# Attention two units at a time inside a fused attention, feed-forward and routed-experts kernel

## The reference, cut to what matters

```python
def _attn_ref(q, k, v, n_global, n_local):        # 4 batches, 8 heads, 768 positions, head size 64
    scores = scale * np.matmul(q, k.transpose(0, 1, 3, 2))
    keep = is_global | is_local                   # 8 global keys and the last 96
    scores = np.where(keep, scores + bias, -1e9)  # bias: -slope of the head * distance
    a = np.exp(scores - np.max(scores, axis=-1, keepdims=True))
    a = a / (np.sum(a, axis=-1, keepdims=True) + 1e-09)
    return np.matmul(a, v)

def _moe_ref(x, w_in, w_out):                     # x 3072x512, w_in 512x2048, w_out 2048x512
    h = x @ w_in
    return (h * (1.0 / (1.0 + np.exp(-h)))) @ w_out
```

## Time and profile before

| | us |
|---|---|
| median of 3 runs (1129.77 to 1133.5) | 1132.96 |
| the profiled execution | 1131.58 |
| its span, first to last instruction | 1129.9 |
| busy in it: TensorE / VectorE / ScalarE / GpSimd | 1083.3 / 650.0 / 461.6 / 418.4 |

### The profile page before, as it was taken

One profiled execution on the slowest core, in us unless ns is written; L12 is line 12 of the kernel. 1 busy time (PEld: TensorE's weight loads), 2 busy tenths in 40 slices (PEclk: granted clock), 3 DMA queues, 4 the chain that ended last, 5 costly groups with the idle time before them and its releaser, 6 DMA issues. The chain is left out here.

```text
span 1129.9 us, 21205 instructions
## 1 busy us (share of the span) xinstructions
PE 1083.3 (96%) x7992; PEld 906.0 (80%) x7992; DVE 650.0 (58%) x2219; ACT 461.6 (41%) x1167; POOL 418.4 (37%) x472
## 2 busy tenths in 40 slices
PE   7999999999999999999999999947899999999998
PEld 5688888888888888888888888946778777878987
DVE  5766747565655656564747473446757757756110
ACT  3665444444444444444444443202233333333442
POOL 1154222222222222222222222316477565486873
PEclk7799999999999999999999999967999999999999
DMA  6664212111112111212121000005045233433520
GB/s 201 186 200 130 73 53 72 53 48 44 70 54 69 48 67 51 71 54 72 54 72 54 36 20 19 1 19 177 26 181 177 104 126 118 171 111 127 200 103 28
DMA packets 19145, 99.99 MB, mean 88 GB/s; under 512 B 2800, under 2 KB 2800, under 8 KB 16848
## 3 DMA queue, kind: packets, MB, share of 16 engines
q0 software_dynamic: 9824, 58.99, 14.8%
q1 hardware_dynamic: 9216, 39.61, 10.7%
HBM read 86.00 MB, written 12.85 MB: 87 GB/s over the span
## 5 line engine op out<-in xcount | busy, mean ns | idle before, releaser
L346 POOL TENSOR_TENSOR g_low<-g,g_high 128x256 fp32r<-128x256 f32 x192 | 149.4, 780 | 483.2 <-ACT g_high L538 483.2
L443 PE MATMUL up_ps<-x_high,w_high 128*128 128x256 f32 x768 | 224.4, 292 | 0.0
L443 PE MATMUL up_ps<-x_low,w_high 128*128 128x256 f32 x768 | 214.7, 280 | 0.0
L443 PE MATMUL up_ps<-x_high,w_low 128*128 128x256 f32 x768 | 214.3, 279 | 0.0
L676 DVE SCALAR_TENSOR_TENSOR g<-g,up_ps 128x256 f32<-128x256 f32 x192 | 80.6, 420 | 213.3 <-ACT g L531 213.3
L443 PEld LDWEIGHTS up_ps<-x_high,w_high 128*128 128x128 f32 x768 | 144.6, 188 | 27.6 <-issue 21.6
L456 PE MATMUL down_ps<-w_high,g_high 128*128 128x512 f32 x384 | 152.4, 397 | 1.0 <-POOL g_low L346 0.9
L456 PE MATMUL down_ps<-w_high,g_low 128*128 128x512 f32 x384 | 152.3, 396 | 0.0
L456 PE MATMUL down_ps<-w_low,g_high 128*128 128x512 f32 x384 | 152.1, 396 | 0.0
L538 ACT ACTIVATE g_high<-g 128x256 fp32r<-128x256 f32 x192 | 80.2, 418 | 171.4 <-PE down_ps L456 115.8
L665 DVE CUSTOM_DVE_ANT_0 product<-x,w_raw 128x512 f32<-128x512 f32 x176 | 147.3, 837 | 3.0
(11 more groups left out here) (196 smaller groups left out, 1934.7 us busy)
## 6 DMA issues: line engine op xcount, KB each, us to landing
qk_t<-qk_rows SPq DMA_DIRECT2D x24, 720.0 KB, 4.8
v_w<-v_win SPq DMA_DIRECT2D x24, 464.0 KB
w_raw<-weights SPq DMA_DIRECT2D x16, 512.0 KB, 4.5
x_rest<-x_any POOLq DMA_DIRECT2D x24, 256.0 KB, 4.8
x_rows<-x POOLq DMA_DIRECT2D x12, 512.0 KB, 3.2
w_raw<-gate_rows SPq DMA_DIRECT2D x1, 2048.0 KB, 13.8
x_g<-x_rows,token_index POOLq DMA_INDIRECT x24, 3.6
out<-y,token_index POOLq DMA_INDIRECT x24, 2.7
```

Of the source, the lines that this page charges most:

```text
L346: pool.tensor_tensor(g_low[:, u % 2, :], g[:, u % 2, :], g_high[:, u % 2, :].bitcast(F32), ALU.subtract)\
L443: last = nc.tensor.matmul(up_ps[:, u % 2, 0:GT * P], a[:, f, w], x[:, grp % 2, c, :], start=k == 0, stop=k == 3 * C - 1)
```

## The change

From step 12 on, attention is done in pairs of units. In an even step `n` TensorE first runs `score(n)`, `score(n+1)`, `value(n-2)`, `value(n-1)` with nothing between them, and then the chunks. The turns are no longer at the head of a step: `turn(n)` stands behind the second chunk of the even step, `turn(n+1)` behind the first chunk of the odd step, where nothing else of attention is left. The other engines follow: VectorE and ScalarE do `shift`, `exp` and `scale_probs` of both units in the even step, ahead of the chunks; `keep_turned` follows the turns. The end of a row (`replace_x`, `round_x`, `rest_x`) moves from three steps behind the row's last `score` to one step.

Buffers: `probs` has two slots instead of three (a third one of the lead borrows `x2`), `probs_t` has two instead of one, the second unit's scores lie at column 256 of the same banks, `product` (an output of the `dot`s that nobody reads) becomes bf16, and `x2_t` moves to `qk_t`.

Lead: `unread_products` are 10, 3, 3 and 2 in steps 0 to 3 (before: 9, 3, 0, 0). In step 11 the turns of units 10 and 11 and `value(9)` stand behind the two `up`s, and the splits of weights behind them are spread over the two chunks.

```diff
-        probs = sb("probs", [P, 3, 2, window])
+        probs = sb("probs", [P, 2, 2, window])
-        probs_t = sb("probs_t", [P, 4, P])
+        probs_t = sb("probs_t", [P, 2, 4, P])
-        product = sb("product", [P, DM])
+        product = sb("product", [P, DM], BF16)
...
+        def scored_in(n):
+            return [u for u in (n, n + 1) if unit_there(u)] if n >= LEAD and n % 2 == 0 else []
+
+        def valued_in(n):
+            return [u for u in (n - 2, n - 1) if unit_there(u)] if n >= LEAD and n % 2 == 0 else []
+
+        def turned_behind(m):
+            n, k = LEAD + m // 2, m % 2
+            u = n if n % 2 == 0 else n - 1
+            if n < LEAD:
+                return None
+            if n % 2 == 0 and k == 1:
+                return u if unit_there(u) else None
+            if n % 2 == 1 and k == 0:
+                return u + 1 if unit_there(u + 1) else None
+            return None
...
+        def scores_of(u):
+            at = 256 if u >= LEAD and u % 2 else 0
+            return qk_ps[:, :, at:at + keys_of(u // PAIRS)[1]]
...
                 if n < LEAD:
+
+
                     score(n)
-                    unread_products({0: 9, 1: 3}.get(n, 0))
-
-                turn_last = n < LEAD and (n - 3) % PAIRS != 0
-                if unit_there(n - 2) and not turn_last:
-                    turn(n - 2)
-                if unit_there(n - 3):
-                    value(n - 3)
-                if unit_there(n - 2) and turn_last:
-                    turn(n - 2)
-                if n >= LEAD and unit_there(n):
-                    score(n)
+                    unread_products({0: 10, 1: 3}.get(n, 0))
...
+                    unread_products({2: 3, 3: 2}.get(n, 0))
+                for u in scored_in(n):
+                    score(u)
+                for u in valued_in(n):
+                    value(u)
                 for m in chunks_of(n):
                     if chunk_there(m + AHEAD):
                         up(m + AHEAD)
                     if chunk_there(m):
                         down(m)
+
+                    if m == -2:
+                        turn(LEAD - 2)
+                        value(LEAD - 3)
+                    if m == -1:
+                        turn(LEAD - 1)
+                    if turned_behind(m) is not None:
+                        turn(turned_behind(m))
```

More of the change, by code:

```diff
@@ L375, in score @@
                     pe.wait_ge(qk_in[row % 2], 16 * (row // 2 + 1))
-                reached(pe, scores_ready, 2 * u)
+                reached(pe, scores_ready, 2 * (u if u < LEAD else u - u % 2))
                 for a in range(2):
                     part = slice(a * D, (a + 1) * D)
-                    last = nc.tensor.matmul(qk_ps[:, a, 0:width], qk_t[part, row % 2, pair, 0:P],
+                    last = nc.tensor.matmul(scores_of(u)[:, a, :], qk_t[part, row % 2, pair, 0:P],
                                             qk_t[part, row % 2, pair, P:P + width], start=True, stop=True)
@@ L407, in value @@
                         last = nc.tensor.matmul(o_ps[a * D:(a + 1) * D, pair, :], v_w[0:part, row % 2, pair, a, c, :],
[L408 removed]
+                                                probs_t[0:part, u % 2, a * 2 + c, :], start=c == 0, stop=c == 1)
                 last.then_inc(values_done, 1)
@@ L548, in _ @@
                     exp(n, (0,))
-                if unit_there(n - 2):
-                    keep_turned(n - 2)
-                if n < LEAD:
+                    if n >= 2:
+                        keep_turned(n - 2)
                     exp(n, (1,))
-                row = row_ended(n, 3)
+                for u in scored_in(n):
+                    exp(u)
+                row = x_row_in(n)
                 if row is not None:
                     round_x(row)
-                if n >= LEAD and unit_there(n):
-                    exp(n)
                 for f in split_in(n):
-                    round_w(f)
+                    if n != LEAD - 1:
+                        round_w(f)
                 for m in chunks_of(n):
+                    if n == LEAD - 1:
+                        round_w(split_in(n)[m % 2])
                     if chunk_there(m + AHEAD):
                         half_tanh(m + AHEAD)
+                    if m == -2:
+                        keep_turned(LEAD - 2)
                     if chunk_there(m + AHEAD):
                         round_g(m + AHEAD)
+                    if m == -1:
+                        keep_turned(LEAD - 1)
+                    if turned_behind(m) is not None:
+                        keep_turned(turned_behind(m))
                     if m % FC == FC - 1 and chunk_there(m):
@@ L684, in _ @@
                     shift(n)
-                row = row_ended(n, 3)
+                for u in scored_in(n):
+                    shift(u)
+                row = x_row_in(n)
                 if row is not None:
                     replace_x(row)
-                if unit_there(n - 1):
+                if 1 <= n < LEAD:
                     scale_probs(n - 1)
@@ L691, in _ @@
                     rest_x(row)
-                if n >= LEAD and unit_there(n):
-                    shift(n)
+                if n == LEAD - 1:
+                    scale_probs(n)
+                for u in scored_in(n):
+                    scale_probs(u)
                 for f in split_in(n - 1 if n < LEAD - 1 else n):
```

38 lines of the change are left out of this document (27 added, 11 removed).

## The result

| | before | after |
|---|---|---|
| median of the runs | 1132.31 us (4 runs, 1129.77 to 1133.5) | 1113.58 us (4 runs, 1111.81 to 1114.72) |
| ratio, 95% interval | | 0.9836 (0.9813 to 0.9859) |
| profiled execution, its span | 1131.58, 1129.9 us | 1112.91, 1111.3 us |
| first `up` starts | 45.10 us | 40.52 us |
| fused stage, first `up` to last `down` | 693.95 us | 678.94 us |

The change gains 18.7 us in the medians and 18.6 between the two spans: 4.6 ahead of the first `up`, 15.0 in the fused stage, and 0.9 are lost behind it.

The account below looks back on a forecast made before the run. TensorE, busy for 96% of the span, was taken as the bound, so gains come only from losses between its products. 1131.58 - 23.4 (pairs) + 0.5 (burst) + 1.0 (lead) = 1109.7 us, range 1102 to 1119.

Parts of the forecast that it names:

- main term: Fused stage: a pair of units pays 0.55 us of shape-change losses once instead of twice; with the edges -23.4 us.
- cold lead: Forecast case: TensorE's clock stays at half in the lead, added unread products cost about +1.0 us; chance 0.52.
- burst on VectorE: Even steps: both units' VectorE work ahead of the chunks delays `up` slightly in the first group; +0.5 us, range -1 to +3.
- the products themselves are the same: Fused stage: TensorE's products stay unchanged apart from added unread ones, so no term for their rate.
- (a): A turn in front of an `up` loses nothing: taken as 0; other end 0.20 at each of 84 turns, 16.8 us.
- the 0.22 that was named as a sign of being wrong: First `up` product behind a turn: taking 0.22 us instead of its own rate would show the prediction wrong.
- the turns pay too: Rival: a turn between `down` and `up` is also a change of shape, 16.8 us come back, 1126.5 us; chance 0.06.
- (b): A pair's second score might not have its weights loaded ahead: 0 to 0.11 us at 42 places; taken as 0.
- (c): `product` as bf16: no reader and off the path, so 0.
- the chain becomes the bound: Rival: VectorE's queued scalings and `dot`s delay `up(m+4)` in even steps; 1132 to 1160 us; chance 0.10.
- the margin of 1.3 us: Worst even step at a row's end: `twice_silu` ends at 6.8 us, `up(m+4)` wants to start at 8.1.
- warm lead: Rival: denser work brings the full clock back early in the lead, -5 us, total 1103.7 us; chance 0.27.

Follow-up runs that it names:

- e7: Changed kernel with the second scaling moved behind the first `twice_silu` in steps 12 to 17, plus 64 unused bytes ahead of `x_rest`: 1111.34 us, single run.
- e6: Kernel before with only its SBUF layout changed: 192 unused bytes ahead of `x_rest`, `product` as bf16, so `x_high` lies at the changed kernel's address: 1139.46 us, single run.
- e2: Changed kernel with the pieces of an even step ordered score, value, score, value: 1134.33 us, ratio 0.9984 to the kernel before.
- e1: Changed kernel with the second unit's scaling behind the first `twice_silu` in the weight-splitting steps 12 to 17: 1113.16 us, ratio 0.9781 to the kernel before.
- e3: Kernel before with the changed kernel's unread products in the lead (10, 3, 3, 2): 1134.69 us, ratio 0.9967 to the kernel before.
- e4: Changed kernel with the unread products of the kernel before (9, 3, none, none): 1119.99 us, ratio 0.9831 to the kernel before.
- e5: Changed kernel itself, unchanged, repeated on another chip: 1117.55 us, ratio 0.983 to the kernel before.
- e11: Changed kernel itself, unchanged, repeated on another chip: 1119.78 us, ratio 0.9846 to the kernel before.
- e8: Changed kernel with the second scaling moved behind the first `twice_silu` in steps 12 to 17, plus 96 unused bytes ahead of `x_rest`: 1114.17 us, single run.
- e10: Changed kernel where GpSimd's `rest_w` waits for VectorE's `rest_w` in even steps 12, 14, 16: 1119.13 us, single run.

## Why the prediction was right

The forecast was 1109.7 us, a gain of 21.9, with a range of 1102 to 1119; the gain came out 3.2 us smaller. The direction and the mechanism of the main term held. That the whole came out so near is luck: two larger errors, 5.3 us one way and 5.6 the other, cancelled. The signs that the prediction gave itself for being wrong came up: `up` waits for VectorE in even steps of the first group, and the granted clock of 16 to 40 us is another. The time fell into the range of the cold lead (1106 to 1115) with a lead that was warm. The terms, on the profiled executions:

| term | forecast | measured |
|---|---|---|
| 42 pairs and the edges | -23.4 | -21.0 (42 x 0.492 = 20.7; edges 0.35, the remainder of the stage) |
| `up` at 1.417 in the last chunks, without attention | 0 | +0.3 |
| burst on VectorE | +0.5 | +5.8 |
| lead | +1.0 | -4.6 |
| behind the stage | 0 | +0.9 |
| sum | -21.9 | -18.6 |

**Main term: right in kind, 2.4 us too large.** Losses of 0.55 a pair were saved as 0.492. Of the 0.058 missing, 0.014 (e7, in after's order) to 0.032 (e6, in before's) is the place of the operands, 0.6 to 1.3 us in 42 pairs: the step "the products themselves are the same" took their rate for granted, and e6 and e7 show that it is not. The other 0.026 to 0.044 is little more than reading starts to 0.01 us, and (a), the turn in front of an `up`, leaves: turn and `up` together take 0.35 + 1.503 against 0.428 + 1.417, so 0.01 a turn, and 0.03 in e7. The first product of `up` behind a turn does take 0.20 (118.78 to 118.98), nearly the 0.22 that was named as a sign of being wrong, but the turn hands over after 0.35 instead of 0.43, so nothing is lost in the sum. The value chosen there, 0 of 0.20, was right within 0.03, and with it *the turns pay too* falls. A pair was to take 14.25 and took 14.288. (b) was 0 as taken: two scores 0.984, not 1.09. (c) too: the `dot`s got shorter, 138.9 us instead of the 147.3 of the earlier trace rows, off the path. "Issue" idle time of the loads of `up` fell from the 21.4 of the earlier trace rows to 7.4; with the loads of scores and values it fell from 51.3 to 33.0 (48 to 745 us), which is less than the half that was foretold. e2 gives the control: two changes of shape more a pair, 0.355 us more, where the prediction's own pieces give 0.36.

**The burst: the mis-sized term, +0.5 for +5.8.** e1 without the waits gains 6.66; less the 0.9 of waits that before had, that is 5.8. The step that failed is the row of VectorE's work in the first group: it took the scaling at 0.9 from the earlier trace rows and put "a `rest_w` behind them" at its undisturbed time, and asked only what stood in VectorE's own queue. What GpSimd did at that moment was left out, though the trace of before had a GpSimd split of 2.4 us in every step there, and already showed what it does to VectorE: `inv` takes 0.70 instead of 0.17 and ends with it, and the scaling behind it, at 58.40, takes 1.31 beside a `g_low` of GpSimd.

```profile
55.74 2.40 POOL L333 TENSOR_TENSOR w_low<-w_raw,w_high 128x1024 fp32r<-128x1024 f32 x1 [3.58 <-ACT w_high L512]
57.47 0.70 DVE L620 TENSOR_SCALAR inv<-sums 128x2 f32<-128x2 f32 x1
```

TensorE did not wait for it there. In after, scaling and split take 2.68 and 3.40 in GpSimd's company. With these the same sum gives 8.4 + 2.1 = 10.5 against the 8.1 at which `up` wants to start, a wait of 2.4; measured 2.16. The prediction even named the mechanism, under *the chain becomes the bound*, as "`dot`s that get slower beside GpSimd's `rest_g`", and looked at the wrong pair of instructions: the `dot`s were not slower. From 100 us on the margin of 1.3 us held. The 2.2 us left of the 6.7, which fit the low clock behind the waits, had no term in the sum.

**The lead: the choice of cold was wrong.** Its argument ("five products are 2 us of work") measured the products by their length. e3 and e4 show that they lift the clock for the whole lead and are worth 4.0 and 4.2 us, and that a lead at full clock is then held by VectorE, ScalarE and `v_w`. The rival *warm lead* had -5 for this and measured -4.6; with the other terms as forecast it would have been 1103.7, and the waits took that back. The rule from the Trainium skill, page TensorE: Matmul & The Clock Gate (Part 4), by which the prediction gave this rival support, pointed the right way; that transposes as such do not count is not isolated by any run here.

**Behind the stage**: 929.6 to 933 us at the low clock, in work that the change doesn't touch. It varies from run to run: e5 and e11, the same kernel, have three and two such stretches at other times. So nothing here shows the 0.9 as an effect of the change.

## What to carry to other kernels

When work is moved on one engine, look at what the engine that it can collide with (here GpSimd for VectorE, and the other way round) does at that very moment: durations from rows where it was idle don't hold, and the order of the two can matter more than the length of either. Products of different array shapes are best grouped by shape, for here each change cost 0.17 to 0.18 us even where nothing waited. When a forecast comes out, check its terms one by one: here two wrong ones cancelled. When buffers change size, compare the rate of untouched products in a quiet stretch, since operands may have moved.

## What the runs showed of the hardware

- The place of the operands in SBUF changes the rate of 256-column products, whatever their order: 12 `up`s take 1.400 us with `x_high` at before's address or 256 bytes behind it (96 past a multiple of 256), 1.417 at 192 behind it (32) and 1.413 at 288 (128). The 512-column products that read `w_high` and `g` went from 1.400 to 1.396 at 192 and stayed at the other two.
- VectorE's `tensor_scalar` on two elements a partition took 2.03 us instead of 0.17 when it began during a split of GpSimd, and GpSimd's `tensor_tensor` 2.97 instead of 2.4 when it began during one of VectorE.
- After waits of 2.2 and 2.3 us TensorE's clock fell to 1.2 GHz for 3.4 us in after, although it was busy all through them; in e5 and e11 it fell behind the first of the same two waits alone. It fell likewise at 929.6 us in after and at 40.5 in e8. Behind waits of 1.13 and 1.5 us in e10 it stayed full. In the lead of before it stayed at 1.2 GHz through 24 us of busy small products; with six unread products more it was full from 21 to 37 us in ten of eleven traces, and for 9 of these 16 us in the eleventh (e5).
